# A branch not taken is rolled up, the first two splits move ahead of the branch, and a join constant moves to PSUM

## The chip, the core and the metric

One core of a Trainium2 chip runs the whole program. Its engines are TensorE (PE), VectorE (DVE), ScalarE (ACT), GpSimd (POOL) and SyncE (SP), which mostly issues transfers. The metric is the device time of one execution in microseconds; lower is better.

## What is computed

Three layers in float32 follow each other: attention with 4 sink keys and a window of 128 (32 heads of 768 rows and 64 columns), a dense layer, and a layer of 8 experts with one expert for each token.

```python
keep = is_sink | in_window            # pos < n_sink, or 0 <= q - k < window
scores = np.where(keep, scale * q @ k.T, -1e9)
a = softmax(scores); attn = a @ v     # q, k, v: (4, 8, 768, 64)
h = x @ w_in; x = (h * cos(h)) @ w_out            # 3072 x 512, 2048 wide
e_idx = argmax(x @ w_gate + modality_bias[modality_id])
out[mask_e] = gate_w * (relu(x @ w1[e]) @ w2[e])  # 8 experts, 1024 wide
```

The window and the number of sinks are inputs, so the kernel must also be right for other values than 4 and 128.

## The kernel before

Each engine has its own instruction stream; the streams meet at semaphores alone. The kernel has three stages: attention (heads taken in 16 pairs, each of `QB = 6` blocks of 128 queries), the dense layer (from about 213 us) and the experts.

There are two ways through the attention. A **narrow path** serves up to 32 sinks and a window of exactly 128, and the inputs timed here take it. A **general path** (`any_pair`, `any_steps`) serves the rest; for these inputs it is code that is jumped over. DVE works out which one from the two inputs (L1021 to L1037) and writes `is_narrow`; every engine waits for `narrow_known`, loads that value into a register and branches (`If(narrow == 0)`, then `If(narrow == 1)`). The branches are at L482 (SP), L635 (POOL), L849 (ACT), L1169 (DVE) and L1617 (PE). In the text of the general path the six blocks of a pair are written out one after the other inside a loop over pairs: on DVE that is, for a block, 7 operations for the mask and 10 for each of two heads, with nearly as many waits, so some 54 instructions a block and some 320 for the six; on ACT some 50 in all, on PE some 200.

On the narrow path the queries and keys of a pair are loaded in four parts (`load_part`, part 0: queries of the first half, 1: keys of the first half, 2 and 3: the second half). SP issues all four for pair 0 at the start, L479. A key part holds two or one copies of the first 32 key columns, the sink keys. Each part is then split in two: ACT rounds it to `hi` (`split_part`, L772), and POOL subtracts to get the rest (`part_rest`, L612; `part_lo_made` counts these). Before a key part is split, POOL overwrites the sink columns past `n_sink` by the first one, with three operations (`fill_sinks`, L606 to L610; `sinks_filled`). For pair 0 all of that comes behind the branch. SP loads a part of the next pair when `part_lo_made` says that the raw tile is free.

A step `n` of the attention is one block of queries. PE makes its scores in `twin[n % 2]`, a tile of two PSUM banks (`scores`, L1507). The first scores wait for two counts: `part_lo_made` 2, and from L1624 and L1625 that DVE has made its masks and the sum columns of V (`make_sink_masks`, `make_sum_columns`, L1047 to L1058, both behind DVE's branch). DVE then joins the scores (`join_scores`): a `copy_predicated` puts, where a mask says so, a second source over the scores (L1073), and a `tensor_reduce` takes the row maxima (L1075). ACT negates the maxima (L783) and exponentiates (L791); PE turns the probabilities two steps later (`turn_probs`, L1527), DVE copies them out (L1083), and PE weighs V with them (L1548). For block 0 of a pair the second source is a constant of -1e30 from the SBUF tile `unseen`; for the others it lies in PSUM, in the same `twin`. Columns 0 to 31 of `twin[1]` hold -1e30 too, set once at L1015, and no product writes there.

## Time and profile before

| | us |
|---|---|
| median of 3 runs | 1096.87 |
| lowest, highest | 1094.04, 1098.3 |
| the profiled execution | 1097.69 |
| its span in the trace | 1095.7 |
| PE busy in that span | 1061.4 (97%) |

| stage | from, us | to, us |
|---|---|---|
| start, up to the first product on PE | 0 | 13.15 |
| attention | 13.15 | 213.75 |
| dense layer and experts | 213.75 | 1095.7 |

The profile is of one execution. A timeline gives for each instruction (or a run of equal ones) its start and its length. The chain of work that ended last is followed back from the end of the program: each piece is what the next one waited for, and "issue" in it is time in which an engine waited for nothing that the profile shows. PEld is the weight load of PE, which overlaps the products. The names with a q (DVEq) are an engine's sequencer. Products on PE are pipelined, so their lengths overlap, and it is their starts that count.

### The profile page before, as it was taken

Reading aid. Unit: us, or ns where it says so; the run is one execution under the profiler, and the core shown is the slowest. Engines: PE = TensorE matmul, PEld = TensorE weight load, DVE = VectorE, ACT = ScalarE, POOL = GpSimd, SP = SyncE. Lnnn points to the kernel's source line nnn. Section 1 sums busy time; section 2 is a strip of 40 time slices with the busy share of each in tenths; the row PEclk is TensorE's granted clock in tenths of the full one; section 3 lists DMA queues with packets and bytes.
Section 4 is the critical chain, followed back from the end, with each engine's and each line's share of the span. In section 5 each row is a group of like instructions: output and inputs, shape, how many; then the busy total and the mean of one; then the engine's idle time right before and its main releaser. Section 6 shows DMA issues by size and latency. Waiting matters only on the chain.

```text
span 1095.7 us, 18853 instructions
## 1 busy us (share of the span) xinstructions
PE 1061.4 (97%) x5976; PEld 915.6 (84%) x5977; DVE 692.9 (63%) x1514; ACT 479.4 (44%) x991; POOL 290.4 (27%) x356
## 2 busy tenths in 40 slices
PE   4999999999999999999999999999999999999997
PEld 4999999878888888888888887888789998999986
DVE  5989999766687578658748768867542222522225
ACT  4878888754433343343334344336341122421124
POOL 6878888700000000000000000511333222222223
PEclk9999999999999999999999999999999999999999
DMA  5877777372120020001002001023261101611102
GB/s 164 258 212 210 209 203 225 108 240 74 77 77 1 1 77 1 1 28 50 1 1 77 1 0 40 5 97 117 88 221 51 46 20 40 192 41 55 37 20 96
DMA packets 58507, 94.90 MB, mean 87 GB/s; under 512 B 11598, under 2 KB 40654, under 8 KB 58320
## 3 DMA queue, kind: packets, MB, share of 16 engines
q1 hardware_dynamic: 52240, 79.76, 23.3%
q0 software_dynamic: 6208, 14.40, 4.0%
q8 instruction: 32, 0.52, 0.2%
q14 instruction: 27, 0.22, 0.1%
HBM read 75.06 MB, written 21.69 MB: 88 GB/s over the span
## 4 chain that ended last, share of the span: by engine, by line
PE 89%; DMA 3%; DVE 3%; issue 2%; ACT 1%; POOL 1%; POOLq 0%; DVEq 0%; ACTq 0%; SPq 0%
PE twin L1650 24%; PE twin L1738 13%; PE bank L1666 12%; PE twin L1666 12%; PE twin L1753 11%; PE bank L1548 6%; PE bank L1527 2%; PE twin L1519 2%; PE twin L1518 2%; PE bank L1555 2%; PE bank L1704 1%; DMA xg<-y_scratch,next_ids 1%; PE bank L1565 1%; DMA out<-late,now_ids 1%; DMA raw_k<-k_twice 1%
## 5 line engine op out<-in xcount | busy, mean ns | idle before, releaser
L690 POOL DMA_INDIRECT list_scratch<-entry,slot_i x24 | 26.7, 1112 | 517.2 <-DVE slot_i L1319 506.0
L1650 PE MATMUL twin<-x_hi,w_hi 128*128 128x512 f32 x384 | 152.6, 397 | 1.4 <-DVE g_sb L1229 0.9
L1650 PE MATMUL twin<-x_hi,w_lo 128*128 128x512 f32 x384 | 152.0, 396 | 0.0
L1650 PE MATMUL twin<-x_lo,w_hi 128*128 128x512 f32 x384 | 151.9, 396 | 0.0
L1440 DVE SCALAR_TENSOR_TENSOR g_lo<-twin,g_hi 128x256 fp32r<-128x256 f32 x112 | 47.5, 424 | 163.2 <-ACT g_hi L948 158.1
L1738 PE MATMUL twin<-xg_hi,w_hi 128*128 128x256 f32 x448 | 127.3, 284 | 2.8 <-issue 2.5
L1738 PE MATMUL twin<-xg_hi,w_lo 128*128 128x256 f32 x448 | 126.0, 281 | 1.2 <-issue 1.2
L1738 PE MATMUL twin<-xg_lo,w_hi 128*128 128x256 f32 x448 | 126.8, 283 | 0.0
L948 ACT ACTIVATE g_hi<-twin 128x256 fp32r<-128x256 f32 x112 | 43.0, 384 | 182.2 <-PE twin L1738 177.1
L912 ACT ACTIVATE turns<-turns 128x512 f32<-128x512 f32 x96 | 60.7, 632 | 134.0 <-DVE turns L1222 132.7
L1204 DVE CUSTOM_DVE_ANT_0 whole<-y_sb,raw 128x512 f32<-128x512 f32 x160 | 109.8, 686 | 1.9
L906 ACT ACTIVATE turns<-twin 128x512 f32<-128x512 f32 x96 | 57.2, 596 | 117.8 <-PE twin L1650 117.6
L1220 DVE TENSOR_SCALAR whole<-turns 128x512 f32<-128x512 f32 x96 | 41.3, 430 | 82.6 <-ACT turns L906 79.9
L917 ACT ACTIVATE g_hi<-g_sb 128x512 fp32r<-128x512 f32 x96 | 60.8, 634 | 72.8 <-DVE g_sb L1229 72.1
L1738 PEld LDWEIGHTS twin<-xg_hi,w_hi 128*128 128x128 f32 x448 | 85.0, 190 | 7.7 <-issue 4.0
L1548 PE MATMUL bank<-v_sb,probsT 128*128 128x65 f32 x704 | 90.4, 270 | 0.1
L1650 PEld LDWEIGHTS twin<-x_hi,w_hi 128*128 128x128 f32 x384 | 72.1, 188 | 20.0 <-DVE g_sb L1229 1.3
L1548 PEld LDWEIGHTS bank<-v_sb,probsT 128*128 128x128 f32 x704 | 87.5, 193 | 0.4 <-DMA v_sink<-v_n 0.3
L1738 PEld LDWEIGHTS twin<-xg_lo,w_hi 128*128 128x128 f32 x448 | 85.1, 190 | 3.2
L1650 PEld LDWEIGHTS twin<-x_hi,w_lo 128*128 128x128 f32 x384 | 72.1, 188 | 17.6
L1738 PEld LDWEIGHTS twin<-xg_hi,w_lo 128*128 128x128 f32 x448 | 85.3, 190 | 1.4 <-issue 1.4
L1650 PEld LDWEIGHTS twin<-x_lo,w_hi 128*128 128x128 f32 x384 | 72.2, 188 | 16.9
(213 smaller groups left out, 2542.7 us busy)
## 6 DMA issues: line engine op xcount, KB each, us to landing
raw<-w_expert SPq DMA_DIRECT2D x32, 512.0 KB, 4.9
raw_q<-q_twice SPq DMA_DIRECT2D x32, 384.0 KB, 3.8
raw<-w_dense SPq DMA_DIRECT2D x16, 512.0 KB, 4.6
raw_k<-k_twice SPq DMA_DIRECT2D x16, 448.0 KB, 3.8
raw_k<-k_twice SPq DMA_DIRECT2D x16, 416.0 KB, 4.7
v_sb<-v_n SPq DMA_DIRECT2D x16, 384.0 KB, 4.1
xT_scratch<-x_stage SPq DMA_DIRECT2D x16, 384.0 KB, 3.8
x_raw<-xT_scratch SPq DMA_DIRECT2D x6, 1024.0 KB, 5.1
```

Source lines behind the costliest of these rows:

```text
L906: act.activation(turns[:, :], H_BANK[f % 2][:, :], ACT.Copy, scale=INV_2PI, bias=0.25).then_inc(turns_made, 1)
L912: act.activation(cosine[:, :], frac[:, :], ACT.Sin, scale=TWO_PI).then_inc(cos_made, 1)
L917: act.activation(g_hi[n % 3][:, :], g_sb[:, :], ACT.Copy).then_inc(g_hi_made, 1)
L948: act.activation(h_hi[f % 4], EH_BANK[f % 2][:, 0:TT], ACT.Relu).then_inc(h_hi_made, 1)
L1204: dve.tensor_tensor_reduce(out=dump[:, :], in0=y_sb[:, t, :], in1=gate_rows[:, e, :], scale=1.0, scalar=0.0, op0=ALU.mult, op1=ALU.add, ac ...
L1220: dve.tensor_scalar(whole[:, :], turns[:, :], ROUND, ROUND, ALU.add, ALU.subtract).then_inc(whole_made, 1)
L1440: dve.scalar_tensor_tensor(out=h_lo[f % 4], in0=EH_BANK[f % 2][:, 0:TT], scalar=0.0, in1=h_hi[f % 4].bitcast(F32), op0=ALU.max, op1=ALU.su ...
L1548: last = pe.matmul(O_BANK[m // 2 % 2][:, at:at + HD + 1], probsT[m % 2][:, b, h, :], v_sb[par][:, i - 1 + b, (HD + 1) * h:(HD + 1) * (h + 1)],
L1650: last = pe.matmul(H_BANK[f % 2][:, :], a[:, w], b[:, k, :], start=x == 0, stop=x == 3 * KD - 1)
L1666: last = pe.matmul(Y_BANK[t][:, :], a[n % 3][:, t * P:(t + 1) * P], b[:, w], start=f == 0 and x == 0, stop=f == FB1 - 1 and x == 2)
L1738: last = pe.matmul(EH_BANK[f % 2][:, 0:TT], a[:, w], b[:, k, :], start=x == 0, stop=x == 3 * KD - 1)
L1753: last = pe.matmul(EY_BANK[j][:, :], a[f % 4][:, j * P:(j + 1) * P], b[:, w], start=f == 0 and x == 0, stop=f == FB2 - 1 and x == 2)
```

## The change

1. The general path is rolled into two loops, over pairs and over blocks, on every engine. For the inputs timed here none of it runs, before or after.
2. For pair 0, the work on parts 0 and 1 comes ahead of the branch and changes engines. ACT issues the load of part 1 itself, runs one exponential on a single column of `ident`, and rounds both parts to `hi` before it branches. DVE does the sink columns of part 1 with one `copy_predicated`, subtracts the two rests (L621's and L623's work) and only then reads `is_narrow` and branches. POOL keeps parts 2 and 3 of pair 0 and everything of the other pairs. SP issues three loads instead of four for pair 0.
3. The tile `unseen` goes. Columns 0 to 31 of both `twin` tiles are set to -1e30, and the join of block 0 takes column 0 of its own `twin` as its second source, spread over the 160 columns.

```diff
@@ sync
+        def load_part(eng, pair, c):      # now outside the streams: SP and ACT call it
-            for c in range(4):
-                load_part(0, c)
+            for c in (0, 2, 3):
+                load_part(sp, 0, c)
@@ gpsimd
-                pool.wait_ge(fill_step, 4 * pair + 2 * half + 2)
+                pool.wait_ge(fill_step, 4 * pair + 2 * half)
...
                 pool.wait_ge(fill_known, 2)
-                for c in range(4):
+                for c in range(2, 4):
                     part_rest(0, 0, c)
@@ scalar
-            def any_pair(pair):
-                for i in range(QB):
...
+            def any_block(pair, i):
+                n = QB * pair + i
...
+            load_part(act, 0, 1)
+            act.wait_ge(consts_made, 4)
+            act.activation(sine[:, :], ident[:, 0:1], ACT.Exp)
+            for c in range(2):
+                split_part(0, 0, c)
             act.wait_ge(narrow_known, 1)
             narrow = act.value_load(is_narrow[0:1, 0:1], min_val=0, max_val=1)
             with act.If(narrow == 0):
...
                 with act.Fori(0, PAIRS) as pair:
-                    any_pair(pair)
+                    with act.Fori(0, QB) as i:
+                        any_block(pair, i)
...
             with act.If(narrow == 1):
-                for c in range(4):
+                for c in range(2, 4):
                     split_part(0, 0, c)
@@ vector
-            dve.memset(unseen[:, :], UNSEEN).then_inc(masks_made, 1)
-            dve.memset(twin[1][:, :, 0:SINK], UNSEEN).then_inc(masks_made, 1)
+            for i in range(2):
+                dve.memset(twin[i][:, :, 0:SINK], UNSEEN).then_inc(masks_made, 1)
...
+            def first_rests():
+
+                to, shape = sinks_of(0), [P, 2, 2, SINK - 1]
+                dve.wait_ge(qk_loaded[1], 16)
+                dve.wait_ge(fill_known, 1)
+                dve.copy_predicated(to[:, :, :, 1:], sink_off[:, 1:].bitcast(U32).unsqueeze(1).unsqueeze(1).broadcast_to(shape),
+                                    to[:, :, :, 0:1].broadcast_to(shape)).then_inc(sinks_filled, 1)
+                for c in range(2):
+                    is_k, cols = part(c)
+                    dve.wait_ge(part_hi_made, c + 1)
+                    if is_k:
+                        dve.tensor_tensor(k_lo[0][:, :, cols], raw_k[:, :, cols], k_hi[0][:, :, cols].bitcast(F32), ALU.subtract).then_inc(part_lo_made, 1)
+                    else:
+                        dve.tensor_tensor(qs[0][HD:, :, cols], raw_q[HD:, :, cols], qs[0][HD:, :, cols].bitcast(F32), ALU.subtract).then_inc(part_lo_made, 1)
+
+            first_rests()
             dve.wait_ge(narrow_known, 1)
             narrow = dve.value_load(is_narrow[0:1, 0:1], min_val=0, max_val=1)
...
                 if i == 0:
-                    into, of, chosen = JOINED, unseen[:, :].unsqueeze(1), masks[:, SINK:]
+                    into, of, chosen = JOINED, to[:, :, 0:1], masks[:, SINK:]
...
                 with dve.Fori(0, PAIRS) as pair:
-                    any_steps(pair)
+                    any_start(pair)
+                    with dve.Fori(0, QB) as i:
+                        any_block(pair, i)
@@ tensor
                 with pe.Fori(0, PAIRS) as pair:
-                    any_pair(pair)
+                    pe.wait_ge(any_loaded, 32 * pair + 32)
+                    pe.sem_inc(carried_pe, 1)
+                    with pe.Fori(0, QB) as i:
+                        any_block(pair, i)
+                    pe.sem_inc(any_free, 1)
```

## Rows read from the trace of the kernel before

**Rows 1.** Chain that ended last, first 20 us (start us, length us, what).

```profile
5.13 0.14 DVEq L1042
...
5.99 5.24 issue
11.22 0.06 DVEq L1179
```

**Rows 2.** Timeline of PE, 13 to 26 us (start us, length us).

```profile
13.15 0.47 PE L1518 MATMUL twin<-k_hi,qs 128*128 128x160 f32 x1 [13.15 <-DVE v_sink L1058]
...
20.59 0.44 PE L1519 MATMUL twin<-k_lo,qs 128*128 128x288 f32 x1
...
25.15 0.29 PE L1519 MATMUL twin<-k_lo,qs 128*128 128x288 f32 x1
```

**Rows 3.** Timeline of POOL, first 17 us.

```profile
10.61 2.08 POOL L621 TENSOR_TENSOR k_lo<-raw_k,k_hi 128x896 fp32r<-128x896 f32 x1 [0.17 <-POOL qs L623]
...
14.13 1.82 POOL L623 TENSOR_TENSOR qs<-raw_q,qs 64x768 fp32r<-64x768 f32 x1 [0.20 <-POOL raw_k L610]
16.11 1.98 POOL L621 TENSOR_TENSOR k_lo<-raw_k,k_hi 128x832 fp32r<-128x832 f32 x1 [0.17 <-POOL qs L623]
```

**Rows 4.** Busy PE, PEld, DVE, ACT, POOL in a stretch; clock, DMA share, GB/s.

```profile
5.00:10.00 5.00, 0.00 (x0) 0.00 (x0) 0.28 (x2) 3.65 (x4) 2.61 (x4) 1.00 1.00 305
...
125.00:150.00 25.00, 25.00 (x199) 23.95 (x198) 23.06 (x57) 20.45 (x59) 20.84 (x22) 1.00 0.72 213
```

**Rows 5.** DMA queues in 10.05:10.1 us: packets, MB, time share.

```profile
q8 instruction: 1, 0.02, 134.9%
```

**Rows 6.** Timeline of ACT, first 9 us.

```profile
6.34 1.28 ACT L779 ACT_TABLE_LOAD   x1 [6.21 <-issue]
7.63 0.84 ACT L779 ACTIVATE qs<-raw_q 128x768 fp32r<-128x768 f32 x1
8.38 0.93 ACT L777 ACTIVATE k_hi<-raw_k 128x896 fp32r<-128x896 f32 x1
```

**Rows 7.** Timeline of SP's issues; the same two transfers, us to landing.

```profile
1.41 0.69 SPq L443 DMA_DIRECT2D raw_q<-q_twice  x1
2.14 0.59 SPq L443 DMA_DIRECT2D raw_k<-k_twice  x1
...
raw_q<-q_twice SPq DMA_DIRECT2D x1, 384.0 KB, 4.0
...
raw_k<-k_twice SPq DMA_DIRECT2D x1, 448.0 KB, 4.5
```

**Rows 8.** DVE groups by shape, first 210 us (busy us, mean ns).

```profile
L1083 DVE TENSOR_TENSOR probsT<-bank,halves_of 128x512 f32<-128x512 f32 x80 | 54.7, 684 | 10.2 <-PE bank L1527 8.9 <-issue 1.2
...
L1073 DVE COPY_PREDICATED twin<-masks,twin 128x320 f32<-128x320 uint32 x16 | 7.8, 487 | 0.0
...
L1083 DVE TENSOR_TENSOR probsT<-bank,halves_of 128x256 f32<-128x256 f32 x16 | 6.6, 414 | 0.8 <-PE bank L1527 0.8
```

**Rows 9.** Line 1073 (ns min/median/max, first and last start); timeline of three joins.

```profile
L1073 DVE COPY_PREDICATED twin<-masks,unseen x16: 567/921/1890, 14.4 to 196.2; 128x320 f32<-128x320 uint32 x16
...
14.41 1.89 DVE L1073 COPY_PREDICATED twin<-masks,unseen 128x320 f32<-128x320 uint32 x1 [1.36 <-PE twin L1519]
...
16.75 0.49 DVE L1073 COPY_PREDICATED twin<-masks,twin 128x320 f32<-128x320 uint32 x1
...
100.91 0.97 DVE L1073 COPY_PREDICATED twin<-masks,unseen 128x320 f32<-128x320 uint32 x1
```

**Rows 10.** Chain, 85 to 109 us: turns of probabilities on PE.

```profile
91.60 0.45 PE bank L1527 x2
...
99.49 0.28 PE bank L1527 x2
...
103.54 0.46 PE bank L1527 x2
```

**Rows 11.** Chain at the last pair, 190 to 200 us.

```profile
196.24 0.81 DVE twin L1073
```

More of the change, by code:

```diff
@@ L143, in build_program @@
             twice_sinks = sb("twice_sinks", [P, 1], where=a)
-            unseen = sb("unseen", [P, WIDE], where=a)
             masks = sb("masks", [P, WIDE + SINK], where=a)
@@ L418, in build_program @@
         T_START, T_END, T_WHOLE, T_EXPERT, T_TILES, T_USED, T_TURNS = 0, 1, 2, 3, 4 * NE + 4, 4 * NE + 5, 4 * NE + 6
+        def load_part(eng, pair, c):
+            is_k, cols = part(c)
+            to, of, width = (raw_k, k_twice, KW) if is_k else (raw_q, q_twice, S)
+            eng.dma_start(to[:, :, cols], of[bass.ds(pair, 1), :, :].rearrange("o p (h s) -> (o p) h s", h=2)[:, :, cols]).then_inc(qk_loaded[c], 16)
         def stage1_over(eng):
@@ L438, in store_chunk @@
                 sp.sem_inc(y_sb_free, 1)
-            def load_part(pair, c):
-                is_k, cols = part(c)
-                to, of, width = (raw_k, k_twice, KW) if is_k else (raw_q, q_twice, S)
-                sp.dma_start(to[:, :, cols], of[bass.ds(pair, 1), :, :].rearrange("o p (h s) -> (o p) h s", h=2)[:, :, cols]).then_inc(qk_loaded[c], 16)
             def load_parts(it, i, cs):
@@ L487, in _ @@
                     sp.wait_ge(any_free, pair + 1)
-                    for h in range(2):
-                        sp.dma_start(any_q[HD * h:HD * (h + 1), h, :],
-                                     q_twice[bass.ds(pair, 1), HD * h:HD * (h + 1), S * h:S * (h + 1)].rearrange("o p s -> (o p) s")).then_inc(any_loaded, 16)
                     sp.dma_start(any_k[:, :], kT[bass.ds(pair, 1), :, :].rearrange("o p s -> (o p) s")).then_inc(any_loaded, 16)
@@ L493, in _ @@
                                  v[bass.ds(pair, 1), :, :].rearrange("o p s -> (o p) s")).then_inc(any_loaded, 16)
+                    with sp.Fori(0, QB) as i:
+                        sp.wait_ge(any_q_free, QB * pair + i + 1)
+                        for h in range(2):
+                            sp.dma_start(any_q[HD * h:HD * (h + 1), h, :],
+                                         q_twice[bass.ds(pair, 1), HD * h:HD * (h + 1), bass.ds(P * i + S * h, P)].rearrange("o p s -> (o p) s"),
+                                         ).then_inc(any_q_loaded, 16)
                 stage1_over(sp)
@@ L635, in _ @@
             with pool.If(narrow == 0):
+                pool.wait_ge(part_lo_made, 2)
                 pool.wait_ge(v_loaded[0], 80)
@@ L1116, in attention, with any_start, any_block @@
                     attention_step(it, n)
-            def any_steps(pair):
+            ANY_BLOCK = 8 + 2 * 7
+            ANY_PAIR = 1 + QB * ANY_BLOCK
+            def any_start(pair):
+                dve.memset(any_at[:, :], 0.0).then_inc(any_step, 1)
+                dve.wait_ge(any_step, ANY_PAIR * pair + 2)
+                dve.sem_inc(carried_dve, 1)
+            def any_block(pair, i):
                 count = [0]
-                per_pair = 7 * QB + 7 * 2 * QB
                 def link(ins):
@@ new lines, in any_block @@
+            def any_block(pair, i):
+                n = QB * pair + i
+                pe.wait_ge(any_q_loaded, 32 * QB * pair + 32 * i + 32)
+                for h in range(2):
+                    u = 2 * QB * pair + 2 * i + h
+                    pe.matmul(bank[0][:, :], any_q[:, h, :], any_k[:, 0:4 * P], start=True, stop=True)
+                    pe.matmul(bank[1][:, 0:S - 4 * P], any_q[:, h, :], any_k[:, 4 * P:], start=True, stop=True).then_inc(any_scored, 1)
+                    pe.wait_ge(any_exp, u + 1)
+                    for g in range(QB):
+                        last = pe.transpose(bank[2 + g // 4][:, g % 4 * P:(g % 4 + 1) * P],
+                                            any_probs[:, g * P:(g + 1) * P], ident[:, :])
+                    last.then_inc(any_turned, 1)
+                    pe.wait_ge(any_copied, u + 1)
+                    for g in range(QB):
+                        last = pe.matmul(bank[4][:, HD * h:HD * (h + 1)], any_probsT[:, g * P:(g + 1) * P],
+                                         any_v[:, g, HD * h:HD * (h + 1)], start=g == 0, stop=g == QB - 1)
+                    last.then_inc(any_weighed, 1)
+                    pe.wait_ge(any_scaled, u + 1)
+                pe.transpose(bank[5][:, 0:P], any_o[:, :], ident[:, :]).then_inc(any_o_turned, 1)
+                pe.wait_ge(any_staged, n + 1)
+                pe.sem_inc(any_q_free, 1)
```

108 lines of the change are left out of this document (45 added, 63 removed).

## Prediction, made before the changed kernel had run

> **What bounds the kernel now.** I read the chain of work that ended last first, cut to the first 20 us. Its longest piece before any product is DVE's: at 5.13 its sequencer starts to load `is_narrow`, at 5.99 it stands at the branch of L1169, and then come 5.24 us of "issue" until L1179 at 11.22 [rows 1]. Nothing is waited for there; DVE only jumps over the general path. Masks and sum columns follow, and PE's first product starts at 13.15, released by them [rows 2]. The second input of that product, the rest of part 1, ends on POOL at 10.61 + 2.08 = 12.69 [rows 3]. So the jump hides a second limit only 0.4 us behind it: a faster jump alone would give 0.4 us.
>
> Then the stretches. In 5 to 10 us the DMA engines are full, share 1.00 at 305 GB/s; in 125 to 150 us PE is busy for 25.00 of 25.00 us and DVE for 23.06 [rows 4]. So the attention is PE's once it runs, with DVE close behind. Of 881.95 us of dense layer and experts the change touches nothing. All that it can give lies in the first 14 us, in the joins of block 0 (16 of them), and in the code's layout.
>
> **DVE's jump.** Why 5.24 us? In the first 9 us no packet of an instruction queue moves; the first one of 16 KB shows in the slice 10.05 to 10.1 [rows 5], behind data that fills the DMA engines [rows 4], and DVE goes on 1.15 us later. That reads as code fetched on demand, queued behind loads. ACT has the same kind of jump, over some 50 instructions and not 320: the same semaphore releases both, so its load of the value starts near DVE's 5.13, and its table load, the first thing behind the branch, starts at 6.34 [rows 6]. That is 1.21 us, of which load and branch would be 5.99 - 5.13 = 0.86 as on DVE; so the short jump costs some 0.35, and 0.5 if ACT was 0.15 sooner. Rolled up, DVE skips some 70 instructions. I take 0.3 us for it (bounds 0.1 and 5.24), by ACT's, the nearest in size. The Trainium skill ("Runtime: NRT & Kernel Launch", Instruction fetch mechanics) says that a taken branch whose target is not in the two resident blocks of 256 instructions waits for a fetch. By that rule 320 instructions leave their own block and 70 need not. The trace agrees with the first half (a 16 KB packet, a stall on DVE alone).
>
> **The work ahead of the branch**, step by step on the clock of the profile. Part 1 (448 KB) is issued at 2.14 by SP and lands 4.5 us later, at 6.64; part 0 at 1.41, landing at 5.41 [rows 7]. ACT can issue part 1 at about 0.96, when SP's stream starts: 1.2 us earlier, landing at 5.4 (bounds 4.9 and 6.6, since the two now share the DMA engines). DVE is through with its constants at about 5.3, just after its sequencer's 5.13 [rows 1].
> - DVE, sink columns: one `copy_predicated` of 124 columns. One of 320 takes 0.49 [rows 8]; I take 0.35: 5.5 to 5.85.
> - ACT: its table load of 1.28 now falls before the data, at about 2 us, in place of 6.34. Rounding starts every 0.75 us and takes 0.84 and 0.93 [rows 6]: queries 5.5 to 6.35, keys 6.3 to 7.2.
> - DVE, rests: a `tensor_tensor` takes 0.414 for 256 columns and 0.684 for 512 [rows 8], so 1.05 ns a column and 0.14 fixed: 0.95 for 768, 1.09 for 896. Queries 6.4 to 7.35, keys 7.35 to 8.45. POOL needed 1.82 and 2.08 [rows 3].
> - DVE's sequencer: 0.86 for load and branch. At 5.13 it ran while the last constant was still being written, so here it should run under the keys' rest, from 7.35 to 8.2; then 0.3 for the jump and 0.13 up to the first mask: 8.65. If it doesn't overlap, 9.75.
> - Masks and sum columns up to PE's first product, before from 11.35 (0.13 behind L1179) to 13.15: 1.80. PE starts at 10.45 instead of 13.15: **-2.7 us** (bounds -3.1, and +3.3 with the full jump and no overlap: 8.45 + 0.86 + 5.24 + 0.13 + 1.80 = 16.5).
>
> Moved past what: SP's three other loads for pair 0, V and the sinks of V go out 0.65 us earlier each. Behind DVE's new waits stand only its masks and sum columns, counted above; behind ACT's, its parts 2 and 3. POOL starts part 3's sinks when `part_lo_made` is 2, at 8.5, if that part, issued near 2.8, has landed (near 9, I estimate); its last rest, 5.4 us of work on, ends near 14.4, was 16.11 + 1.98 = 18.09 [rows 3]. PE is in the products of its fourth block, which need it, at 20.59 [rows 2], 7.4 us after its start, 6 with the shorter join: about 16, 1 to 1.5 us to spare. Pair 1's loads go out some 3 us earlier. `unseen`'s memset lies in a wait for the configuration: nothing.
>
> **The join of block 0.** With `unseen` it takes 0.57 to 1.89 us, median 0.92, in 16 cases; the same shape out of `twin` takes 0.487 in the mean of 16 [rows 8, 9]. The reason stands in two timelines. The first join (14.41 to 16.30) ends just after POOL's `tensor_tensor` of 14.13 to 15.95; the next, with its source in PSUM, starts at 16.75 in the middle of POOL's 16.11 to 18.09 and takes 0.49 [rows 3, 9]. So a join with two SBUF sources waits until POOL is through, one with a single SBUF source doesn't. The Trainium skill ("SBUF — State Buffer", Who interferes with whom) says the same: a DVE instruction with two SBUF inputs contends with a GpSimd one that reads SBUF. Now each term:
> - First join: on the path, since PE and ACT have nothing else to do. 1.89 to 0.49: **-1.4** (bounds -1.3 and -1.4).
> - Middle pairs: the row maximum comes earlier by 0.97 - 0.49 = 0.48 at every second pair, by 0.09 at the others. PE's turn of those probabilities takes 0.46 in the chain after a long join, 0.45 after a short one, an ordinary one 0.28 [rows 10]. So 0.18 a pair is there to be won; a long join's 0.48 covers it, a short one's 0.09 may be lost in the steps between. 7 long ones at 0.18: **-1.3** (bounds 0 and -2.7, 15 pairs).
> - Last pair: the join is in the chain with 0.81 [rows 11] and would take 0.49: **-0.3** (bounds 0 and -0.4; ACT's weight splits come right behind).
>
> PE runs at the lower of its two clock levels (1.2 GHz) at first: a product of 288 columns is put at 0.44 us at 20.59 and at 0.29 at 25.15 [rows 2], 0.15 less for 288 columns, though the granted clock reads 1.00 throughout. I shift the rise with the start; if it comes 2 us earlier or later relative to the work, that is 1 us either way.
>
> **Sum:** -2.7 - 1.4 - 1.3 - 0.3 = -5.7. The profiled execution took 1097.69, so 1092.0. It lies 0.8 above the median of the three runs (1096.87), so against the median 1091.2. I forecast between the two: 1091.5, or 5.4 to 5.7 us less (0.5%).
>
> **Rivals.**
> 1. *The jump stays.* Its price is in the fetch, not in the distance: the target is fetched on demand either way. For: nothing in the trace shows DVE jumping cheaply. Against: ACT's 0.5. DVE is at the masks at about 13.6 (8.2 + 5.24 + 0.13), PE starts at 15.4: +2.25, and with the joins' -3.0 it is -0.75: 1096.5. Chance 0.15.
> 2. *The middle pairs give nothing*, since PE is full and the 0.18 are its own order, and the overlap on DVE or the landing costs 1 us: -2.7 + 1 - 1.4 = -3.1: 1094.2. For: PE's 25.00 of 25.00 [rows 4], and the 0.45 after a short join. Chance 0.30.
> 3. *Slower: the code's new layout hits a loop.* DVE's stream loses some 240 instructions ahead of the attention loop and PE's some 160. If a loop that now fits comes to lie so that its code is fetched again in each of its 7 turns, a turn costs at least the 1.15 us between the packet and DVE's going on, 8 us, and up to 5.24, 37 us, while DMA is busy. 1091.5 + 8 = 1099.5 and more. It decides against the change from 0.8 us a turn. Against: DVE's loop is only some 100 instructions by the code, and the trace shows DVE busy for 23.06 of 25.00 us in it [rows 4], with no room for such a gap. Chance 0.07.
> 4. *The change to PSUM doesn't act* (a single column spread over 160 reads slower than a row): the joins stay near 0.9, the sum is -2.7: 1094.2. Chance 0.05.
>
> My forecast, with all four terms, has 0.43.
>
> **How the numbers follow.** About 0.5% (5.5 us) is what a measurement of this kernel can tell from no change. The forecast sits right at that line: of its 0.43, 0.27 fall on the faster side and 0.16 within; of rivals 1, 2 and 4 (0.50) a tenth spills to faster, 0.05, through the clock's 1 us and the joins' wider bound; rival 3 splits into 0.05 slower and 0.02 within. So faster 0.32, same 0.63, slower 0.05. The forecast's own range is 1089.0 to 1093.5. The wider one takes in rivals 1, 2 and 4, the best bounds (-3.1, -1.4, -2.7, -0.4 and 1 for the clock: 8.6 below the median, 1088.3) and most of the first rival's spread: 1088.0 to 1097.3.
>
> **What would show it.** Right: DVE's chain has no "issue" above 0.5 us behind the branch; PE's first product at 10 to 11 us; POOL's first operation is L606's for part 3; the first join at 0.5; no join of block 0 above 0.55 in any pair; PE's turns after block 0 at 0.28 in the chain. Wrong: a gap of several us on DVE after the branch, a 16 KB packet just before it ends; part 1 landing after 6; the joins of block 0 spread as now; new idle time on PE at about 15 or 22 us, which would mean POOL's rests come late; gaps of "issue" at the head of each turn of the attention loop.

## The result

The changed kernel takes 1100.6 us in the median of 9 runs (1096.49 to 1103.69), the kernel before 1095.7 in 9 runs beside it (1094.04 to 1098.35): a ratio of 1.0040, 95% interval 1.0024 to 1.0056. It is slower by 0.4%, where 0.5% less was forecast, and lies outside the range. The profiled execution spans 1099.7 us, that of before 1095.7.

The time did not go where the change was made. The two timelines side by side, at points that both have:

| point | before | after | difference |
|---|---|---|---|
| PE's first product | 13.15 | 11.91 | -1.2 |
| first `x_stage` copy (ACT, L806, now L812) | 28.5 | 25.5 | -3.0 |
| eighth of the 48 copies | 57.00 | 53.15 | -3.9 |
| last copy, the attention's end | 213.30 | 207.88 | -5.4 |
| first second-layer product of the dense layer (L1666, now L1705) | 223.45 | 222.7 | -0.7 |
| PE at its branch in the expert stage, first of 3 executions (L1803, now L1842) | 787.3 | 789.3 | +2.0 |
| rounding of the last gathered tokens (ACT, L896, now L907) | 923.72 | 924.88 | +1.2 |
| PE at the same branch, last execution (the "late branch") | 1069.1 | 1068.7 | -0.4 |
| PE's last product | 1088.96 | 1092.91 | +4.0 |

So the attention is 5.4 us shorter, close to the 5.7 of the forecast. What follows gives back 9.4 us. By 787 us 7.4 are lost, and 4.4 more behind PE's late branch. In between the kernel before loses 2.4 net against the changed one: 0.8 between 787 and 812 us, and 1.6 behind 924, where it has the lower clock for 3.4 us from 928.3. PE runs the same 5976 products in both kernels. Compared one by one, the difference of their starts goes from -5.4 to -0.7 at 223 us of before, where PE of the changed kernel idles, to +1.95 by 227, where it has the lower clock, and stays within 0.02 of that until 777. So the first loss is 4.7 + 2.7 = 7.4 us and lies wholly at the head of the dense layer.

**The start**, the chain that ended last (start us, length us, what), answering [rows 1], and the first product:

```profile
1.41 5.34 DMA raw_q<-q_twice
...
9.46 0.53 issue
...
10.98 0.85 DVE v_sink L1085 x8
11.82 0.09 issue
11.91 0.47 PE twin L1553
```

DVE's 5.24 us behind the branch are 0.53. The head of the chain is now the load of part 0's queries, which land 5.34 us after their issue, at 6.75; before it was 4.0 [rows 7]. The lower clock of the start ends at 20.4 us instead of 23.8, which is 3.4 us earlier, while the first product is only 1.2 us earlier.

**The rests on DVE and the first join** (timeline), and the joins of all pairs (ns, min/median/max), answering [rows 3] and [rows 9]:

```profile
7.64 0.96 DVE L1065 TENSOR_TENSOR qs<-raw_q,qs 64x768 fp32r<-64x768 f32 x1 [1.40 <-ACT qs L785]
8.63 1.09 DVE L1063 TENSOR_TENSOR k_lo<-raw_k,k_hi 128x896 fp32r<-128x896 f32 x1
...
13.18 0.50 DVE L1100 COPY_PREDICATED twin<-masks,twin 128x320 f32<-128x320 uint32 x1 [1.36 <-PE twin L1554]
...
L1100 DVE COPY_PREDICATED twin<-masks,twin x96: 419/429/497, 13.2 to 200.9; 128x256 f32<-128x256 uint32 x64, 128x320 f32<-128x320 uint32 x32
```

No join takes above 0.50 us any more; the first one took 1.89.

**First loss, the head of the dense layer.** The chain of after from 208 to 223 us:

```profile
208.29 4.15 DMA xT_scratch<-x_stage
...
212.75 7.50 DMA raw<-w_dense
...
220.28 1.06 ACT w_hi L776
...
221.36 1.24 DVE w_lo L1129
...
222.74 1.62 PE twin L1705 x3
```

In before no transfer stands in this part of the chain. There the store of the last staged x was issued at 213.71 and landed 2.4 us later; the next weights were asked for at 216.39, 2.7 us after the store was issued, and PE found them ready (issue of the store with us to landing, then SP's timeline):

```profile
xT_scratch<-x_stage SPq DMA_DIRECT2D x1, 384.0 KB, 2.4
...
216.39 3.71 SPq L467 DMA_DIRECT2D raw<-w_dense  x4
```

Here it is 4.46 us from the store to the weights, although the same wait stands between them in both kernels. Why the store is slow shows in the DMA queues of the changed kernel, from 209.0 to 209.1 us and from 210.3 to 212.1 us (packets, MB, time share):

```profile
q8 instruction: 1, 0.02, 100.8%
...
DMA packets 9, 0.02 MB, mean 14 GB/s; under 512 B 1, under 2 KB 1, under 8 KB 9
...
q1 hardware_dynamic: 9, 0.02, 4.7%
```

One packet of 16 KB of PE's code starts at 209.07 and takes 1.61 us on one of the 16 DMA engines, so until 210.68. The store's other packets are through by 210.25. Its last nine come one after another from 210.67 until 212.0: 4.7% of 16 engines is less than one engine's 6.25%, and the first of them starts when the code's packet is through. So I take them to have waited behind it on its engine; the trace doesn't number the engines. SP waits for the whole store before it asks for four parts of the dense weights. POOL's 1.5 MB of `list_scratch` stores, which in before came behind the first two of these loads (216.98), now go out ahead of them (211.56).

**PE and its clock** in three stretches (us, busy, granted clock, DMA share, GB/s), first of before, then of after:

```profile
215.00:221.00 6.00, 5.09 (x22) 1.00 0.67 224
221.00:228.00 7.00, 7.00 (x31) 1.00 1.01 392
...
1069.00:1080.00 11.00, 9.27 (x69) 1.00 0.38 115
```

```profile
215.00:221.00 6.00, 3.06 (x12) 1.00 0.99 341
221.00:228.00 7.00, 5.26 (x13) 0.56 1.04 264
...
1069.00:1080.00 11.00, 7.37 (x38) 0.69 0.20 58
```

PE does 25 products instead of 53 in 215 to 228 us: first it idles 4.6 us, then it has the lower of its two clock levels (granted 0.56 in the mean, 1.2 GHz for 6.8 us from 221.8).

**Second loss, PE's late branch.** The chain of after, and PE's branch in the records of before and after (ns, min/median/max of its 3 executions):

```profile
1068.94 3.69 issue
1072.63 7.15 PE twin L1777 x36
```

```profile
L1803 PEldq COMPARE_BRANCH  x3: 65/86/425, 787.3 to 1069.1; - x3
...
L1617 PEldq COMPARE_BRANCH  x1: 6597/6597/6597, 6.0 to 6.0; - x1
```

```profile
L1842 PEldq COMPARE_BRANCH  x3: 65/86/3553, 789.3 to 1068.7; - x3
```

The last of the three took 425 ns before and 3553 ns after, with no semaphore waited for. The chain of before at this place:

```profile
1069.32 0.57 issue
1069.88 1.55 PE twin L1738 x11
1071.44 1.17 issue
1072.61 3.23 PE twin L1738 x25
```

So before has 0.57 and 1.17 of "issue" there and the 36 products in 4.78 us; after has 3.69 and 7.15, at the lower clock for 6.8 us from 1071.7. That is 1.95 + 2.37 = 4.3 us. What the branch waits for shows in the instruction packets beside it: in after one is through at 1068.2 and the next runs from 1069.74 to 1070.88, and the branch ends at 1072.24, 1.36 us behind that second packet. The row of L1617 is the one that I had not looked for: PE's own first branch took 6.6 us in before, from 5.99 to 12.59, and ends 1.4 us behind a packet of 10.09 to 11.17.

The diff touches nothing at either place. What it did change there is where the code lies: PE's program has 8043 instructions instead of 8493, so everything behind the general path moved up by 450. PE's instruction queue (q8) moves 31 packets of 16 KB, 0.51 MB, in the profile's queue table, some 30 us apart in the dense layer. I take a packet to be one of the blocks of 256 instructions that the prediction speaks of; the runs with 0 and with 256 instructions of padding test that.

### The profile page after: what moved, and what is told of

It reads as the page before. It is cut to its first block, busy times and chain, and to the rows that moved or that the text cites. A ratio compares the mean times of both kernels' runs of the same rounds, so it can differ in the third digit from the quotient of the medians.

```text
span 1099.7 us, 18850 instructions
## 1 busy us (share of the span) xinstructions
PE 1063.9 (97%) x5976; PEld 918.9 (84%) x5977; DVE 690.4 (63%) x1517; ACT 480.3 (44%) x992; POOL 280.9 (26%) x351
## 4 chain that ended last, share of the span: by engine, by line
PE 91%; DMA 3%; DVE 2%; issue 2%; ACT 1%; POOL 1%; DVEq 0%; POOLq 0%; SPq 0%; ACTq 0%
PE twin L1689 24%; PE twin L1777 14%; PE twin L1792 12%; PE bank L1705 12%; PE twin L1705 12%; PE bank L1583 6%; PE bank L1562 2%; PE twin L1554 2%; PE twin L1553 2%; PE bank L1590 2%; PE bank L1743 1%; PE bank L1600 1%; DMA raw<-w_dense 1%; DMA raw_k<-k_twice 1%; DMA raw_q<-q_twice 0%
```

## The experiments

My theory after the result: **the place of PE's code within its blocks of 256 instructions** makes both losses, by a fetch that falls on the last store and by a late branch whose target is not there yet. "Place" below is the size of PE's program modulo 256. The rival: the attention's earlier end makes a race of transfers at 208 us (the place of the code plays no part), and the late branch follows from it. Padding is the tool: dead semaphore increments at the head of PE's general path, which the narrow path jumps over (N of them, from here on "dead instructions").

```
                 pe.sem_inc(any_free, 1)        # in the general path
+                for _ in range(N):
+                    pe.sem_inc(carried_pe, 1)
```

### The join alone

The kernel before with `into, of, chosen = JOINED, to[:, :, 0:1], masks[:, SINK:]` and the columns of `twin[0]` set too.

> The kernel before with the third part of the change alone: both twin tiles get -1e30 in columns 0 to 31, the join of block 0 takes its constant from there. No instruction stream changes its length. Layout theory (the loss of the change comes from where PE's code blocks of 256 instructions end): PE's blocks lie as before, so the attention gets shorter by the joins and nothing is given back: first join 0.50 us instead of 1.89, first dense product 3 to 4 us sooner than 213.75, no PE wait near 222, ratio 0.996 to 0.998. Race theory (the dense layer's weight loads fall behind GpSimd's list stores just because the attention ends sooner): the same wait of 4 to 5 us near 220 as after the change, ratio 1.000 or above.

1093.31 us, ratio 0.9970 (0.9960 to 0.9981). The first join takes 0.497 us. Its gain of 3.1 us answers the forecast's -1.4 - 1.3 - 0.3 = -3.0. The attention ends 3.5 us sooner (last `x_stage` copy at 209.77), PE does 53 products in 215 to 228 us as in before, and the late branch takes 0.48 us: with PE's code in its old place an earlier end alone makes neither loss.

### PE's general path as before

```
-                    with pe.Fori(0, QB) as i:
-                        any_block(pair, i)
+                    any_pair(pair)          # 6 blocks written out
```

> The changed kernel, with the general path of PE alone written out as before (it isn't run for these inputs). PE's code is then 8499 instructions of 64 bytes instead of 8043, and 6 more than before, so its code blocks end where they did before. Layout theory: PE's branch in the expert stage takes 0.4 us and not 3.55, the last store of the attention lands in 2.4 us and not 4.1, PE does not wait 4.6 us at the start of the dense layer; PE's first branch again takes several us, so its first product stands at 12.5 to 13.2. Ratio to before 0.994 to 0.997 (about 1091). Race theory: the wait at the start of the dense layer stays; ratio 1.000 to 1.004.

1091.55 us, ratio 0.9964 (0.9947 to 0.9981): 8499 instructions, all other parts of the change kept. PE's first branch takes 5.46 us again, yet ends at 12.1 and costs only 0.5 at the start (first product at 12.44). The late branch takes 420 ns, and the store at the attention's end lands in 2.4 us. Rolling PE's path alone turns a gain of 0.4% into a loss of 0.4%.

### 120 and 40 dead instructions

> The changed kernel with 120 more semaphore increments inside PE's general path, which isn't run. Nothing else differs; the target of PE's first branch moves from instruction 205 to 325. Layout theory: the time moves by some us in either direction against the changed kernel (1.004), since each later block ends 120 instructions (about 14 us of dense work) sooner; the block fetched at 209.1 us moves to about 195; and PE's first branch becomes slow again (several us) since its target leaves the first block of 256. Race theory: ratio 1.004 as the changed kernel, the same wait near 220.

1088.51 us, ratio 0.9930 (0.9912 to 0.9949). The same stretches as above:

```profile
215.00:221.00 6.00, 5.34 (x22) 1.00 0.94 335
221.00:228.00 7.00, 7.00 (x31) 1.00 1.02 302
1069.00:1080.00 11.00, 11.00 (x77) 1.00 0.49 166
```

Code that never runs makes the changed kernel 12 us faster: 53 products in 215 to 228 us as in before, the late branch 756 ns, and the granted clock nowhere at the lower level from 19.4 to 1084 us. The race of transfers is refuted: the attention ends nearly as early here (208.5 for 207.9), and PE finds its weights ready. Two parts of the expectation failed. The packet of 209.1 us went to 203.7 and not to about 195. And PE's first branch, whose target went from instruction 205 to 325, took 0.37 us and not several.

> The changed kernel with 40 more semaphore increments inside PE's general path, which isn't run: the target of PE's first branch moves from 205 to 245, still in the first 256. Layout theory: PE's first branch stays short (under 0.5 us), the block fetched at 209.1 us is fetched at about 204, so the last store lands in 2.4 us, SP's weight loads go out some 1.7 us sooner, and the wait of 4.6 us goes; the expert stage's branch may be short or long. Ratio 0.994 to 1.001. Race theory: 1.004.

1094.64 us, ratio 0.9990 (0.9976 to 1.0004). The fetch is off the store (205.2 us) and the first loss is gone, while the late branch still takes 3340 ns. The two losses are separate.

### The kernel before, padded

> The kernel before with 15 further semaphore increments at the head of TensorE's general path: 8508 instructions of TensorE instead of 8493, and nothing else changed. The work of every stage is the same. Theory (TensorE's code is fetched in blocks of 16 KB over the same DMA engines as the data, and the result of the change is set by where the blocks fall): the block's packet that landed at 216.3 us moves some 1.7 us earlier, onto the last store of the transposed x; that store then takes about 4 us instead of 2.4, the later dense weights are asked for some 1.7 us later, TensorE waits 4 to 5 us near 223 us and gets the lower clock after it. Ratio 1.004 to 1.007. Rival (code layout plays no part in this wait; it comes from the earlier end of attention alone): ratio 0.999 to 1.001 and no wait near 223 us.

1098.04 us, ratio 1.0022 (1.0013 to 1.0031). The mechanism that I expected did not come: the code's packet started at 216.0 (216.3 in before), not 1.7 us earlier, and PE did not wait near 223. But the late stall did grow, just behind the branch, in the chain:

```profile
1070.65 2.64 issue
```

This stall lies among the products, with no branch in it, and ends 1.5 us behind a packet of 1070.39 to 1071.78; so it is a fetch too. 15 instructions that never run cost 0.2%. I can't place a fetch in time from the count of instructions; I can only say which place repeats which.

> The kernel before with 62 further semaphore increments in TensorE's general path: 8555 instructions of TensorE, that is those of the changed kernel (8043) and two blocks of 256, so the code behind the general path lies in its blocks of 256 instructions (16 KB) exactly as in the changed kernel; everything else is that of the kernel before. Theory (the place of the code in its blocks decides): TensorE's branch near the end of the expert stage takes about 3.5 us instead of 0.43, with a stall and the lower clock behind it, some 4 to 5 us; if the block's packet also falls on the last store, 4 to 6 us more at the dense layer. Ratio 1.004 to 1.008. Rival (something else of the rolled code, not its place): the branch stays at 0.4 us, ratio 0.999 to 1.002.

This one repeats the place of the changed kernel in the kernel before (8555 = 8043 + 2 x 256). 1105.04 us, ratio 1.0080 (1.0061 to 1.0099). Both losses are there, in the chain and in the branch:

```profile
213.49 3.42 DMA xT_scratch<-x_stage
...
217.23 5.55 DMA raw<-w_dense
...
1068.85 3.47 issue
...
L1805 PEldq COMPARE_BRANCH  x3: 65/89/3322, 789.4 to 1068.6; - x3
```

Not one part of the change is in this kernel, and it loses twice what the change lost. Its late branch ends 1.40 us behind the packet of 1069.60 to 1070.53.

### The changed kernel at the place of before, and one block further

> The changed kernel with 194 increments in TensorE's general path: 8237 instructions, that is those of the kernel before (8493) less one block of 256, so the code behind the general path lies in its blocks as in the kernel before. Theory: no wait near 222 us, the late branch of the expert stage at 0.4 us, all of what the change earns is kept: 1089 to 1091 us, ratio 0.993 to 0.996. Rival (the place of the code does not decide): ratio 1.000 to 1.004.

1090.86 us, ratio 0.9954 (0.9940 to 0.9968). 8237 = 8493 - 256; the late branch takes 605 ns, no wait at 222 us.

> The changed kernel with 256 increments in TensorE's general path, one whole block of 16 KB: 8299 instructions, the same places within the blocks as in the changed kernel, a longer jump at the start. Theory (place within the block): the branch of the expert stage takes 3.5 us again and the lower clock follows, and the slow last store is back as well; ratio 1.002 to 1.005. Rival (any added code helps, since it is the length of the jump or the total size that counts): ratio 0.993 to 0.996, as with 120 increments.

1100.59 us, ratio 1.0034 (1.0020 to 1.0048), the changed kernel's own 1.0040 within the interval:

```profile
208.54 4.09 DMA xT_scratch<-x_stage
...
L1844 PEldq COMPARE_BRANCH  x3: 65/86/3306, 789.0 to 1070.7; - x3
```

Here too the store's last packets start when the code's packet is through (210.82 for 210.83). 120 instructions heal it, 256 bring all of it back. It is not how much code there is but where in a block it lies. All kernels by their place:

| place | kernels | late branch, us | slow last store |
|---|---|---|---|
| 45 | before, the join alone, changed + 194 | 0.43, 0.48, 0.61 | no |
| 51 | changed, PE's path as before | 0.42 | no |
| 60 | before + 15 | 0.42, then a stall of 2.64 | no (2.9) |
| 107 | changed, changed + 256, before + 62, changed with early loads | 3.55, 3.31, 3.32, 3.47 | 4.15, 4.09, 3.42, 4.1 |
| 147 | changed + 40 | 3.34 | no |
| 227 | changed + 120 (two executions), before + 182, the five edits below | 0.76, 0.75, 0.58, 0.42 to 0.86 | no |

In the four kernels of place 107 and in changed + 40 the late branch ends 1.34 to 1.48 us behind a packet that started only after PE had reached the branch; in the others it is through before PE gets there.

### The weights ahead of the store

SP issues dense weights 4 to 7 before `stage1_over` and its wait for the last stores; PE's code is unchanged.

> The changed kernel, but SP issues the parts 4 to 7 of the dense weights (in the narrow path) ahead of its wait for the last stores, so that these loads no longer stand behind the slow store. TensorE's code is unchanged. Theory (two separate stalls): the wait of 4.6 us near 222 us and the lower clock behind it go, some 6 us in all; the stall of 3.6 us at TensorE's branch near 1069 us and its lower clock stay. Time about 1094.5 us, ratio about 0.999. Rival 1 (the fetch of the code itself starves TensorE near 222 us, not the late weights): the stall stays in another form, ratio 1.003 or more. Rival 2 (the earlier loads collide with the store and delay the transposed x): a new wait at the dense layer's start, ratio 1.001 to 1.004.

1094.6 us, ratio 0.9988 (0.9979 to 0.9997), 6 us better than the changed kernel. The store is as slow as ever (first row, us to landing), but nothing stands behind it; the late stall stays (second row):

```profile
xT_scratch<-x_stage SPq DMA_DIRECT2D x1, 384.0 KB, 4.1
...
1062.56 3.61 issue
```

So the first loss is worth some 6 us in the medians, with its clock (7.4 in the traces of before and after), and an order of SP's queue cures it without padding. What is left of the change's loss is the second one; it keeps this kernel about level with the one before.

### What each part of the change is worth

All at the place of 120 (227), so that the place of PE's code is the same in all of them.

> The changed kernel with 120 further increments in TensorE's general path (1088.51 us, ratio 0.993), and VectorE's inner loop over the blocks of the general path written out again, so that VectorE's branch jumps over 8 blocks' code; VectorE has 2058 instructions instead of 1794. Theory (the jump over much code costs the engine some us): VectorE idles about 5 us behind its branch as in the kernel before, the masks and the first join come some 4 us later, TensorE starts at 15 to 16.5 us instead of 11.9; ratio 0.996 to 0.997. Rival (the jump is only as slow as the DMA traffic beside it, and VectorE now branches earlier than in the kernel before): the stall is below 2 us, ratio 0.993 to 0.994.

VectorE's inner loop written out again. 1091.72 us, ratio 0.9968 (0.9955 to 0.9981). The stall is back, in the chain:

```profile
9.54 4.20 issue
```

PE's first product starts at 15.65 instead of 11.94, so DVE's short jump is worth 3.7 us at the start. In the time it is less sure: 0.9968 against 0.9930 and 0.9946 of the same kernel without this edit, some 2.4 to 4.2 us.

> The changed kernel with 120 further increments in TensorE's general path (1088.51 us, ratio 0.993), without the part of the change that splits the first two parts ahead of the branch: ScalarE and GpSimd split them behind it, as in the kernel before. Theory (the splits ahead of the branch earn the 1.2 us by which TensorE started earlier): GpSimd's first rests end at about 12.5 us, TensorE's first product starts at about 13.1 instead of 11.9, ratio 0.994. Rival (TensorE's own jump and the masks set the start just as well): first product within 0.4 us of 11.9, ratio 0.993.

Splits behind the branch on ACT and POOL, as in before. 1090.74 us, ratio 0.9960 (0.9947 to 0.9973). The theory's sign is right and its size too small: the first product comes 1.75 us later (13.69), and the first `x_stage` copy 3.1 later (28.45 for 25.34), because POOL has four rests of the first pair to do and not two. In the chain PE waits 1.39 us, until 27.82, for ACT, whose work stood behind POOL's sink columns of a later part. I had priced this part by its first product only.

> The kernel before with 182 further semaphore increments in TensorE's general path: 8675 instructions, those of the changed kernel with 120 increments (8163) and two blocks of 256. So the kernel before stands at the place in the blocks that served the changed kernel best. Theory (the place decides a part, the change the rest): the late branch takes below 0.9 us, no wait near 222 us, the drops of the clock from 928 us on go; 1.5 to 4 us less than before, ratio 0.9965 to 0.9985; the changed kernel at the same place (0.993) is then 4 to 5.5 us better, which is what the change by itself is worth. Rival (before was already at a place with no loss): ratio 0.999 to 1.001.

The kernel before at that place: 1094.31 us, ratio 0.9987 (0.9978 to 0.9996). The place gives the kernel before 0.13%.

> The changed kernel with 120 increments in TensorE's general path once more, for the comparison with the two others of this job: ratio 0.992 to 0.995.

1089.91 us, ratio 0.9946 (0.9933 to 0.9960). Against the kernel before at the same place, on the same chip, the change by itself is worth 1094.31 - 1089.91 = 4.4 us. Two more pairs at equal places, both measured on one other chip, say much the same: 1105.04 - 1100.59 = 4.5 at place 107, and 1096.35 (before, unpadded) - 1090.86 = 5.5 at place 45.

### The masks ahead of the branch

```
+            make_sink_masks()
+            make_sum_columns()
             first_rests()
             dve.wait_ge(narrow_known, 1)
...
             def narrow_attention():
-                make_sink_masks()
-                make_sum_columns()
```

> The changed kernel with 120 increments in TensorE's general path (ratio 0.993), and VectorE makes the sink masks and the sum columns (12 small instructions, 10.12 to 11.8 us in the changed kernel, the last thing that TensorE's first product waits for) ahead of its branch, in the idle time before part 0's queries land at 6.8 us. Theory (the start is now set by these masks): TensorE's first product starts 1.4 to 1.7 us earlier, at about 10.3 us; ratio 0.9915 to 0.992, some 1.5 us better. Rival (TensorE's own path or the rests end just as late): first product within 0.5 us of 11.9, ratio 0.993.

1089.36 us, ratio 0.9942 (0.9929 to 0.9955). The first product is 2 us earlier, and its releaser is now the rest itself:

```profile
9.97 0.47 PE L1553 MATMUL twin<-k_hi,qs 128*128 128x160 f32 x1 [9.97 <-DVE k_lo L1063]
```

Its ratio overlaps that of 120 increments alone (0.9930 on another chip), so the two ran again on one chip.

> The changed kernel with 120 increments, and VectorE's sink masks and sum columns ahead of its branch, once more, beside the same kernel without that move. Theory (the first product's 2 us are kept to the end, as in its trace, where the last product came 2.1 us earlier): 1.5 to 2.1 us below pad120_again. Rival (the 2 us are lost in later waits in most executions): within 0.7 us of it.

1087.62 us, ratio 0.9920 (0.9907 to 0.9932), the lowest median here, 2.3 us below 1089.91 on the same chip. That looked like the theory; the next pair did not repeat it.

### Who issues part 1

```
-            for c in (0, 2, 3):
+            for c in range(4):
                 load_part(sp, 0, c)
...
-            load_part(act, 0, 1)
```

> The changed kernel with 120 increments in TensorE's general path, and SP issues part 1 right behind part 0, as the kernel before does, instead of ScalarE beside them at 0.96 us; the splits stay ahead of the branch. Theory (part 1's loads beside part 0's are what delays part 0: it lands 5.3 to 5.7 us after its issue in all kernels with the new order and 3.9 to 4.1 in all with the old one, the configuration after 3.0 to 3.4 instead of 2.5 to 3.1): part 0 lands 4.0 us after its issue, VectorE's first rest starts 1.3 us earlier, at about 6.4, but the keys' rest waits for part 1, which lands at 6.6 or 6.7; TensorE's first product at about 11.1 instead of 11.9 us, and a time 0 to 0.8 us below that of 120 increments alone (1088.5 to 1089.9), ratio 0.992 to 0.995. Rival (the landing has another cause, such as the table load): part 0 lands after 5.3 us again and the first product does not move or comes later.

1090.30 us, ratio 0.9946 (0.9933 to 0.9960). Part 0 in this kernel, and in the one with 120 increments alone (us to landing, the last number):

```profile
raw_q<-q_twice SPq DMA_DIRECT2D x1, 384.0 KB, 3.8
```

```profile
raw_q<-q_twice SPq DMA_DIRECT2D x1, 384.0 KB, 5.4
```

The order of issue is the cause: 3.8 to 4.1 us in eight kernels with the old order, 5.3 to 5.7 in nine with the new. But the first product moves only to 11.65. VectorE's sink columns need part 1 and stand ahead of its first rest, so the queries that land at 5.2 wait for the keys' load:

```profile
6.84 0.30 DVE L1056 COPY_PREDICATED raw_k<-sink_off,raw_k 128x124 f32<-128x124 uint32 x1 [1.55 <-DMA raw_k<-k_twice]
```

> The same, and VectorE's sink masks and sum columns ahead of its branch. Theory: VectorE is through with the masks at about 7.2 us, then the rests of queries and keys, 2.1 us, and the branch: first product at 9.5 to 9.9 us, no more than 0.5 us ahead of the same kernel with part 1 from ScalarE (9.97), since the masks now fill the time that the earlier landing frees; ratio 0.991 to 0.994. Rival: the first product at 9 us or below.

1089.85 us, ratio 0.9940 (0.9927 to 0.9954), first product at 9.47. Against 1090.30 on the same chip that is 0.5 us for a first product 2.2 us earlier. Over three pairs of runs the kernels with the masks moved have 1089.36, 1087.62 and 1089.85, those without 1088.51, 1089.91 and 1090.30. In this pair's traces the first `x_stage` copy starts at 24.3 instead of 25.0, the eighth at 52.95 instead of 53.12. So in this pair most of the head start is gone within three pairs of heads. Not in every trace: `pad120_masks_first` ends the attention at 207.26, 1.2 us ahead of the 208.47 with 120 dead instructions alone, `pad120_masks_again` at 208.62 for 208.45. I don't count the move as a gain. The fastest kernel that holds up is the changed one with 120 increments, 0.993 and 0.9946 of the time before; it beats both kernels.

## Why the prediction was wrong

Point by point, by its own steps.

- **"Of 881.95 us of dense layer and experts the change touches nothing"**: this is the step that failed. All of the 9.4 us that were given back lie there. The work there is the same, but its instructions have to be fetched too, over the DMA engines that carry the data, and 450 instructions fewer shift each fetch. The term that was put at nothing measured 8.7 and 9.7 us: 1105.04 for 1096.35 in the kernel before, 1100.59 for 1090.86 in the changed one, for place 107 instead of 45. The count was wrong too: I had PE lose some 160 instructions of a general path of some 200, and it lost 450.
- **Rival 3, the new layout** (0.07), had the right suspect with the wrong mechanism and the wrong place: a fetch repeated in each turn of the attention loop, from 8 us on. Measured were single events: one packet on one store (some 6 us by the run with early loads), and one jump (4.3 us by the chain). No gap stands at the head of the loop's turns. I had argued the rival away by looking at loops alone; the durations of PE's own branches in the trace of before would have given 6.6 us for one jump, and the late one (0.43 us beside 0.07 and 0.09) as the next candidate.
- **The packet of [rows 5]** was misread. I took the 16 KB of 10.05 us for DVE's code and the stall for DVE's alone. It is PE's: padding PE's path alone moves the packets of that queue (209.1, 205.2 and 203.7 us with 0, 40 and 120 dead instructions), and PE stood in a branch of its own until 12.59, 1.4 us behind that packet. The other engines' instruction queue moved packets of 8 KB at 9.12 and 9.45 us. The second shows in the stretch of 9.4 to 9.6 us of before; it is through at 9.89, and DVE goes on 1.33 us later:

```profile
q14 instruction: 1, 0.01, 13.8%
```

  So that DVE's long jump waits for a fetch still stands, and the 0.3 us for the short one, which came from ACT, isn't touched. But the 1.15 us on which rival 3 built its 8 us do not measure one engine's wait.
- **The start** was -2.7 and measured -1.24. DVE's parts were right: sink columns 0.30 for 0.35, rests 0.96 and 1.09 for 0.95 and 1.09, jump and first mask 0.66 from 9.46 to 10.12 for 0.43, overlapped with the rest as assumed, masks and sums 1.79 for 1.80. The mis-sized term is the landing of part 0, 5.34 us after its issue and not 4.0. I had the two loads share the DMA engines and gave the bound to part 1 alone (which landed at 5.6 for 5.4); the one that paid was part 0, 1.34 us. So DVE's first rest starts 1.24 us later than forecast (7.64 for 6.4), and the jump up to the first mask takes 0.23 more: together the 1.5 us that were missing.
- **The first join**: -1.39 for -1.4. **The middle pairs**: from the eighth to the last `x_stage` copy 154.73 us instead of 156.30, so -1.57 with the last pair in it, for -1.3 and -0.3. No join is above 0.55. PE's turns after block 0 are not at 0.28, though, but at 0.31 to 0.40 in the chain. **The last pair**: the join in the chain is 0.42 for 0.49. Rivals 2 and 4 are out.
- **Rival 1, the jump stays**: out, 0.53 us. The other way round, with DVE's path written out, it is 4.20. The Trainium skill ("Runtime: NRT & Kernel Launch", Instruction fetch mechanics) says that a taken branch out of the two blocks at hand waits for a fetch. PE's first branch agrees: with its target at instruction 655 (205 + 450, worked out from the two sizes) or further it took 5.5 to 7.0 us, with one at 325, 399 or 461 it took 0.37, and at 205 or 245 0.24 and 0.23. At the same place the Trainium skill calls the cost of going on into the next block mostly hidden; here the packets of the dense layer bear that out (between 227 and 777 us PE loses nothing by them against before), but the one beside the last store cost some 6 us, and in the kernel before with 15 dead instructions PE stood for 2.64 us, among its products, until one had come.
- **PE's own jump**, 5.99 to 12.59, was missing from the list of limits behind the first product of before. It lay 0.56 us behind the first product, and the rolled PE path takes it away; left in, it costs 0.5 us. That my start was not further off for it is luck.
- **The sum** for the attention, -5.7, measured -5.4, and that is partly luck. The start gave 1.5 us less than forecast, and yet the eighth `x_stage` copy is 3.85 us earlier, where start and first join together give 2.63 and the joins of the next pairs 0.18 each by the prediction's own price. What fits the rest is the clock: the lower level lasts from 11.9 to 20.4 us instead of from 13.15 to 23.8, 2.1 us less, which the prediction priced at about 1 us either way. No run shows that the change makes the clock rise sooner against the work. Without its placement the change is worth 4.4 to 5.5 us, near the forecast's 5.7 or a fifth below it. Inside the attention the terms held but for the start; what the forecast had wrong is the path behind it.
- **Rival 4's** time doesn't follow from its sum: -2.7 gives 1094.6, not 1094.2. Nothing hangs on it.

What stays open: how much of a start earlier than 11.9 us reaches the end; and which instruction's passing starts a fetch, and so at what moment a packet lands; the run with 15 increments shows that I can't compute it. Nor was it tried to move the late branch alone.

## What to carry to other kernels

When an edit changes the number of instructions of an engine, even in a path that never runs, list the long branches of that engine and the instruction packets beside them before and after: they are a term of the sum. Look also at the packets beside stores and loads that something waits for. A result within 1% of such an edit says little until the same edit has been run with a few different paddings; here the same change gave 0.993, 0.995, 0.999, 1.003 and 1.004. And a wait for a store that stands ahead of loads which don't need it makes a single slow packet expensive: issue those loads first.

## What the runs showed of the hardware

- A packet of 16 KB of code took 0.9 to 2.2 us (599 packets in 19 traces, median 1.0). In the changed kernel the last nine packets of a store came only when one of them was through, 1.75 us behind the others.
- An engine that had to wait for its code went on 1.3 to 1.5 us after the packet was through: PE at its first branch in six traces and at the late branch wherever that took over 0.5 us, DVE at its long jump in before.
- PE's jumps at the expert stage's branch took 0.07 to 0.09 us in the two earlier executions and 0.42 to 0.86 or 3.3 to 3.6 us in the last; from up to 0.5 us before the end of a stall of 2.6 us and more there to 2 us behind it, PE's clock fell to the lower level, for 3.4 or 6.8 us.
- VectorE's jump over some 320 instructions took 5.24 us, while PE's over more than 256 (the padding alone) took 0.37. The packets of the other engines' instruction queue are of 8 KB (26 of 0.21 MB in the profile of after), half of PE's.
- `copy_predicated` of 320 columns with mask and source in SBUF took 0.57 to 1.89 us, each of the 16 beside a `tensor_tensor` of GpSimd; with the source in PSUM it took up to 0.50. The Trainium skill ("SBUF — State Buffer", Who interferes with whom) says that a VectorE instruction with two SBUF inputs contends with a GpSimd one that reads SBUF, and that with at most one, outside its two-port modes, it doesn't; the traces agree.
